# Start addresses of the long SBUF tiles set to multiples of 2048 bytes, with the odd row of tokens placed last, in a fused attention and feed-forward kernel

## What is computed

```python
# attention: a causal band of n_local = 96 keys, and the first n_global = 8 keys
scores = where(keep, scale * q @ k.T - slope[h] * dist, -1e9)
x = softmax(scores) @ v                      # [2, 768, 512]
# first network: mixing over tokens of rank 32, then 512 -> 2048 -> 512
u = x + ((x.T @ U) @ V).T
x = u + maximum(u @ w_ch1, 0) @ w_ch2
# second network, on each token and the one before it
xk = mu_k * x + (1 - mu_k) * x_prev
xr = mu_r * x + (1 - mu_r) * x_prev
k = maximum(xk @ w_k, 0)                     # 512 -> 1024
out = sigmoid(xr @ w_r) * ((k * k) @ w_v)    # 1024 -> 512
```

## The kernel before

| tiles | before | after |
|---|---|---|
| ident | 128 | 128 |
| weights of both slots, raw, XRH, XRL, x_nat | 1216 | 0 |
| UH, UL, Y | 1216 | 0 |
| HH, HL, WVH, WVL, WRH, WRL, here, ahead, q_in, k_in | 1248 | 0 |
| v_in, v_rest, probs, probs_t | 2016 | 768 |
| VH4, A4 / VL4 | 1984 / 960 | 768 / 1792 |

## Time and profile before

### The profile page before, as it was taken

How to read it: one execution, slowest core, us unless ns; L and a number is a source line. 1 busy time by engine, 2 the same in 40 slices (tenths; PEclk the granted TensorE clock), 3 DMA queues, 4 the chain that set the end, 5 groups by cost and what they waited for, 6 DMA issues and landing times.

```text
span 527.9 us, 9725 instructions
## 1 busy us (share of the span) xinstructions
PE 515.8 (98%) x3824; PEld 423.8 (80%) x3824; DVE 183.3 (35%) x479; ACT 131.0 (25%) x352; POOL 242.5 (46%) x228
## 2 busy tenths in 40 slices
PE   4899999999999999999999999999999999999997
PEld 4788888888888888888888888888888788888885
DVE  5777775121312213123131331312444333331323
ACT  4777874111101001010110001121322132203220
POOL 3254657164009000089600829980899479960000
PEclk9999999999999999999999999999999999999999
DMA  6867745104002200024400000000000200020002
GB/s 215 294 222 225 250 162 188 47 0 160 0 0 81 79 0 0 0 79 160 159 0 0 0 0 0 1 0 1 0 1 0 80 0 0 0 79 0 0 0 79
DMA packets 15344, 33.84 MB, mean 64 GB/s; under 512 B 1488, under 2 KB 1872, under 8 KB 15312
## 3 DMA queue, kind: packets, MB, share of 16 engines
q1 hardware_dynamic: 14736, 32.57, 18.2%
q10 hardware_dynamic: 576, 0.84, 0.5%
HBM read 30.25 MB, written 3.15 MB: 63 GB/s over the span
## 4 chain that ended last, share of the span: by engine, by line
PE 97%; DVE 1%; DMA 1%; issue 0%; POOL 0%; ACTq 0%; POOLq 0%
PE psum L574 26%; PE psum L562 25%; PE psum L627 13%; PE psum L618 12%; PE psum L642 6%; PE psum L421 5%; PE psum L433 3%; PE psum L455 3%; PE psum L447 1%; PE psum L463 1%; PE psum L473 1%; DVE probs L855 1%; PE psum L470 1%; DMA k_in<-in_k 1%; PE psum L471 1%
## 5 line engine op out<-in xcount | busy, mean ns | idle before, releaser
L970 DVE SCALAR_TENSOR_TENSOR HL<-psum,HH 128x512 fp32r<-128x512 f32 x48 | 33.2, 692 | 175.0 <-ACT HH L754 175.0
L754 ACT ACTIVATE HH<-psum 128x512 fp32r<-128x512 f32 x48 | 28.7, 598 | 234.1 <-PE psum L562 234.1
L574 PE MATMUL psum<-HH,w2h 128*128 128x512 f32 x192 | 76.3, 397 | 0.0
L574 PE MATMUL psum<-HL,w2h 128*128 128x512 f32 x192 | 75.9, 395 | 0.0
L574 PE MATMUL psum<-HH,w2l 128*128 128x512 f32 x192 | 75.7, 394 | 0.0
L562 PE MATMUL psum<-UH,w1h 128*128 (+1 forms) x192 | 75.6, 394 | 0.0
L562 PE MATMUL psum<-UL,w1h 128*128 (+1 forms) x192 | 75.0, 391 | 0.0
L562 PE MATMUL psum<-UH,w1l 128*128 (+1 forms) x192 | 74.7, 389 | 0.0
L1092 POOL TENSOR_SCALAR w1h<-raw 128x2048 fp32r<-128x2048 f32 x4 | 7.7, 1915 | 121.6 <-PE psum L574 121.6
L673 ACT ACTIVATE probs<-probs,neg_max 128x192 f32<-128x192 f32 x96 | 42.5, 444 | 19.8 <-DVE neg_max L855 19.6
L1009 DVE TENSOR_TENSOR k_square<-k_relu 128x512 f32<-128x512 f32 x24 | 22.5, 938 | 68.3 <-ACT k_relu L779 68.2
(11 more groups left out here) (118 smaller groups left out, 883.6 us busy)
## 6 DMA issues: line engine op xcount, KB each, us to landing
v_in<-in_v SPq DMA_DIRECT2D x16, 384.0 KB, 4.7
raw<-in_moe_w_ch SPq DMA_DIRECT2D x6, 1024.0 KB, 5.3
v_rest<-in_v_rest SPq DMA_DIRECT2D x8, 384.0 KB, 3.6
out<-result SPq DMA_DIRECT2D x12, 256.0 KB, 2.1
k_in<-in_k SPq DMA_DIRECT2D x7, 432.0 KB, 4.2
q_in<-in_q SPq DMA_DIRECT2D x7, 384.0 KB, 3.2
raw<-in_moe_w_ch SPq DMA_DIRECT2D x8, 256.0 KB, 4.3
raw<-in_moe_w_v SPq DMA_DIRECT2D x2, 1024.0 KB, 5.1
```

What stands on the lines that cost most here:

```text
L574: mm = pe.matmul(bank[d][:, 0:BLK], w[:, f, d * P:(d + 1) * P], x[:, f % 2, :], start=f == 0 and n == 0, stop=f == FQ - 1 and n == 2)
L754: act.activation(HH[:, f % 2, :], bank[4 + f % 2][:, 0:BLK], ACT.Relu).then_inc(hid_high, 1)
L970: dve.scalar_tensor_tensor(out=HL[:, f % 2, :], in0=bank[4 + f % 2][:, 0:BLK], scalar=0.0, in1=HH[:, f % 2, :].bitcast(F32), op0=ALU.max, ...
```

## The change

Three long regions are rounded up to a multiple of 2048 bytes at their start: the weights of slot 0 (and so all that follows them), and UH behind the largest of the tiles that share x_at. Y goes from between UL and HH to the end, behind `ahead`. Its rows are of odd length still. No instruction, wait or shape changes, and each engine has the same instructions in the same order.

```diff
+        LINE = 2048
+
         class Region:
             def __init__(self, start):
                 self.at = start
+
+            def align(self):
+                self.at += -self.at % LINE
...
         mu_rest = fixed("mu_rest", [P, 2, KT])
+        fixed.align()
         wq_names = ("w1h", "w1l", "w2h", "w2l")
         slot0 = [fixed(n + "_0", [P, 4, QF], F32R) for n in wq_names]
...
         A4 = region("A4", [P, 2, P], F32R)
+        region.align()
         y_at = region.at
...
         UH = region("UH", [P, KT, TOK], F32R)
         UL = region("UL", [P, KT, TOK], F32R)
-
-        Y = region("Y", [P, KT, TOK + 1])
         h_at = region.at
         HH = region("HH", [P, 2, BLK], F32R)
...
         here = region("here", [P, BLK])
         ahead = region("ahead", [P, BLK])
+
+        Y = region("Y", [P, KT, TOK + 1])
         end = region.at
```

## The result

| | before | after |
|---|---|---|
| median of 6 runs | 529.93 us (528.43 to 534.58) | 521.25 us (520.89 to 522.76) |
| ratio, 95% interval | | 0.9839 (0.9812 to 0.9867) |
| profiled execution | 529.68 us | 522.44 us |
| its span | 527.9 us | 520.7 us |
| TensorE busy | 515.8 us | 508.3 us |

The account below looks back on a forecast made before the run. TensorE, busy 98% of the span, was taken as the bound. Savings of 4.8, 2.2 and 0.3 us, 7.3 in all, gave 522.4 us from the profiled run and 523.5 from the median; 523.0 was forecast, range 508 to 531.

Parts of the forecast that it names:

- If every long interval is the settled one: Long matmuls of both feed-forward networks: all take 0.2267 us each, where the slow lines L574 and L642 took 0.2333.
- The sum: Both networks: 4.8, 2.2 and 0.3 us saved, 7.3 us in all; span from 527.9 to 520.6 us.
- the first step: First network, first pair of quarter and block: pieces of L574 and L562 lose 0.07 + 0.15 + 0.06, 0.3 us.
- the eleven others: First network, remaining pairs of quarter and block: 21.76 us each in place of 22.20, 4.8 us saved in all.
- the three blocks: Second network, gate, keys and values: 54.40 us a block in place of 55.12, 2.2 us saved in all.
- Attention and the first transfers at 0: First 90 us: transposes (at most 3.6 us possible) and the q_in and k_in transfers (bounded by 0.5 us) taken as 0.
- The cover of GpSimd: Second network, j = 1: GpSimd's last result precedes the keys by 9.4 us; TensorE takes back 0.7 in a block.
- 32 bytes apart: L574 and L642: moving and next stationary operands start 32 bytes apart, giving 0.2333 us where equal residues give 0.2267.
- neither 1216 nor 1248 is slow in itself; the two together are: Long matmuls: equal starts modulo 2048 settle at 0.2267 or 0.227 us, one operand at each start at 0.2333.
- A: Long matmuls: starts themselves count, multiples of 2048 bring up to 25.0 us more, 497.4 us or 498; chance 0.14.
- B: L574 and L642: addresses don't matter, they are slow for another reason, time stays 529.7 to 530.8 us; chance 0.12.
- C: Every long matmul: at residue 0 all take 0.2333 us, 4.7 us slower, 534.4 or 535.5 us; chance 0.08.

Follow-up runs that it names:

- the padded kernel: 224 bytes of padding behind Y and nothing else, against the kernel before the change: 521.83 us, ratio 0.9833.
- the first two experiments: Y last, nothing aligned, against the kernel before: 522.39 us, ratio 0.9858; Y back between UL and HH, starts aligned, against the changed kernel: 529.80 us, ratio 0.9993.
- the second kernel of the last experiment: HL, XRL and WVL put at 32 modulo 256, other tiles left at 0, against the changed kernel: span 526.3 us, one run.

## Why the prediction was right

**The interval.** "If every long interval is the settled one" was the step on which the sum rested, and it held to the digit: 2.72, 5.44, 8.16, 10.88. A step went from 22.20 to 21.76 (136.66 to 158.42), a block's gate, keys and values to 54.40 us (354.26 to 408.66).

**The sum.** 7.3 us were forecast, 7.4 came from the networks, and 7.2 in the span: 520.7 for 520.6. By parts, the first step lost 0.2 us (24.68 to 24.45) where the sum had 0.3, the eleven others 4.8 as forecast, and the three blocks 0.9, 0.7 and 0.7. So the 0.1 between 7.3 and 7.4 is the first block, which the sum had counted as one of 55.12: it took 55.30, most of it in its last piece, where the other blocks have 8.19 and 8.20 for 36 values.

```profile
405.96 8.36 PE psum L627 x36
```

As to the median, 521.25 for 523.0. The gap is in the run times of before, whose median was 530.82 over 3 runs and 529.93 over 6, and in the changed kernel's profiled run, which was 1.2 us above its median. Taken from the median of 6, the sum gives 522.6. The 1.4 us that are left are in no term of the sum, and the run times of either kernel spread over more than that.

**Attention and the first transfers at 0.** The numbers were right: 0.81 and 0.33 us again, and landings 0.1 earlier. The reasons were weaker. That probs and the identity would agree after the change holds modulo 64 and not modulo 256, so the 0 tested nothing; and in no run here do they agree modulo 256. That transposes in float32 don't mind the distance is not shown. Nor does the time of twice the bytes bound what another start costs a transfer; that the landings moved by 0.1 us is the evidence. The networks start at 90.15 us before, 90.45 after, 88.66 in the padded kernel and up to 91.69 in the other kernels without narrowed matmuls, so a span from one profile is uncertain by more than a microsecond for reasons ahead of the networks.

**The cover of GpSimd.** Right: TensorE never waited for it. The cover fell by 1.5 us, not 0.7: TensorE took back 0.9, as this stretch lies in the longer first block, and the shift took 0.7 longer in this run.

**The cause.** The part that said "32 bytes apart" was right: the first two experiments part it from alignment cleanly. Two details of it were wrong. The period isn't 64, which its paragraph on attention had, but 256 bytes. And that "neither 1216 nor 1248 is slow in itself; the two together are" is true also of mixes of 0 and 32 in which each moving operand agrees with the stationary one after it.

**The rivals.** A (starts as such) would have shown L562 under 2.70; with Y last and nothing aligned it has the same 2.72 at 1216, and no start or distance gave less. B is refuted by the gain itself, and the two independent read ports of the Trainium skill's page "TensorE: Matmul & The Clock Gate" (section "Step-by-step: what each phase is for"), on which it leaned, don't make the interval independent of addresses: the runs have 0.2267 to 0.236 for one shape. Nor did the 215.7 ns that the Trainium skill gives on the same page (section "Wait — 56ns, not 53.3ns?") come back at any distance tried for this type: the least was 226.7. C fell with 2.72 at residue 0.

## What to carry to other kernels

Where TensorE is never idle, compare the length of a chain piece over its count between lines of the same shape: a difference of 3% is a cost per matmul, and here it was the tile addresses. Keep the starts of all operands of long fp32r matmuls (128x128 stationary, 512 columns moving, as measured here) a multiple of 256 bytes apart, those of neighbouring lines too; a tile of odd length in their midst breaks it for all that follow, and a few bytes of padding behind it mend it. Test such a theory by moving one tile alone before writing down which alignment is needed: here the edits that looked like the change did nothing, and the one that looked like tidying did all.

## What the runs showed that I had not expected

- The relation has a memory. Behind L574, a line at another residue, L562 took seven to nine intervals until it was settled:

```profile
114.67 0.39 PE L562 MATMUL psum<-UH,w1h 128*128 x1
...
116.28 0.39 PE L562 MATMUL psum<-UH,w1l 128*128 x1
...
119.91 0.39 PE L562 MATMUL psum<-UL,w1h 128*128 x1
...
136.86 0.40 PE L562 MATMUL psum<-UH,w1h 128*128 x1
...
138.94 0.39 PE L562 MATMUL psum<-UH,w1h 128*128 x1
```

  These are starts in the timeline of before. In the piece from 114.67 the first 7 intervals take 1.61 us, 0.230 each, the next 16 take 3.63, 0.2269 each. In the next step's, from 136.86, the first 9 take 2.08 us, 0.231 each, and so do those of the piece from 270.06. Not every slow line leaves this behind it, as the second kernel of the last experiment shows.
- How dear a distance is doesn't grow with it: 72 and 240 bytes are the dearest tried (2.82 and 2.83 for 12), 64 the least dear (2.76).
- Matmuls whose stationary operand has 32 columns in place of 128 run at a longer interval, 2.78 for 12, and unsettle the full ones behind them (5.47 for 5.44).
- At best 32 cycles stay over the 512 columns. No distance tried took them away; what they are stays open, as does the mechanism of the 256 bytes.
